# Attention and two feed-forward layers on one core: attention moved ahead of the first layer, which then runs in blocks of 1024 tokens by seven half-size products

## The reference

```python
# decaying linear attention: batch 4, 8 heads, 768 steps, head size 64
state = gamma * state + k[t] (x) v[t];   y[t] = scale * q[t] @ state
# first feed-forward (512 -> 2048 -> 512)
h = x @ w_in;  g = where(h > 0, h, exp(min(h, 0)) - 1);  x2 = g @ w_out
# second feed-forward (512 -> 1024 -> 512)
h = x2 @ w_in2; e = exp(h - max(h)); solu = h * e / (sum(e) + 1e-9)
out = (layer_norm(solu) * g_ln) @ w_out2
```

## Time and profile before

| | us |
|---|---|
| median of 3 runs | 891.65 |
| the profiled execution | 891.52 |
| its span in the trace | 889.7 |
| TensorE matmul busy | 880.3 (99%) |
| VectorE busy | 447.5 (50%) |
| ScalarE busy | 327.6 (37%) |
| GpSimd busy | 182.1 (20%) |

### The profile page before, as it was taken

The page is one execution under the profiler, slowest core; times in us unless marked ns, Lnnn a source line. Parts: engine busy times, 40 slices in busy tenths (PEclk is TensorE's granted clock), DMA queues, the critical chain, the costliest instruction groups (busy, mean ns, idle before and its releaser), DMA issues.

```text
span 889.7 us, 12234 instructions
## 1 busy us (share of the span) xinstructions
PE 880.3 (99%) x4998; PEld 718.4 (81%) x4998; DVE 447.5 (50%) x755; ACT 327.6 (37%) x524; POOL 182.1 (20%) x214
## 2 busy tenths in 40 slices
PE   8999999999999999999999999999999999999998
PEld 6788888888888888888888888888878888888886
DVE  4765433332333333332333233376797777777774
ACT  2654433233333333333333335553243333333332
POOL 4221102110111102110110015330334444444200
PEclk9999999999999999999999999999999999999999
DMA  9901131110301122110310021410211111111001
GB/s 346 407 26 45 48 93 50 48 49 1 122 21 48 48 65 78 48 48 1 97 46 1 1 71 48 144 47 1 71 49 47 48 48 48 48 48 48 24 25 47
DMA packets 34007, 57.81 MB, mean 65 GB/s; under 512 B 2848, under 2 KB 15392, under 8 KB 33952
## 3 DMA queue, kind: packets, MB, share of 16 engines
q1 hardware_dynamic: 33376, 56.70, 18.1%
q10 hardware_dynamic: 576, 0.33, 0.1%
HBM read 44.44 MB, written 12.58 MB: 64 GB/s over the span
## 4 chain that ended last, share of the span: by engine, by line
PE 95%; DVE 3%; issue 1%; DMA 0%; POOL 0%; ACT 0%; POOLq 0%; DVEq 0%; ACTq 0%
PE ps L508 11%; PE ps L512 10%; PE ps L486 10%; PE ps L509 10%; PE ps L487 10%; PE ps L492 10%; PE ps L609 4%; PE ps L611 4%; PE ps L610 4%; PE ps L520 4%; PE ps L522 4%; PE ps L521 4%; PE ps L440 3%; PE ps L471 3%; PE ps L595 2%; PE ps L468 1%
## 5 line engine op out<-in xcount | busy, mean ns | idle before, releaser
L734 DVE TENSOR_TENSOR g_lo<-e,g_hi 128x512 fp32r<-128x512 f32 x96 | 74.3, 774 | 168.3 <-ACT g_hi L967 168.1
L508 PE MATMUL ps<-g_hi,w_hi 128*128 128x512 f32 x384 | 154.0, 401 | 0.0
L486 PE MATMUL ps<-x_hi,w_hi 128*128 128x512 f32 x384 | 149.5, 389 | 0.7 <-ACT x_hi L924 0.7
L512 PE MATMUL ps<-g_lo,w_hi 128*128 128x512 f32 x384 | 149.9, 390 | 0.0
L509 PE MATMUL ps<-g_hi,w_lo 128*128 128x512 f32 x384 | 149.6, 390 | 0.0
L487 PE MATMUL ps<-x_hi,w_lo 128*128 128x512 f32 x384 | 149.4, 389 | 0.0
L967 ACT ACTIVATE g_hi<-e 128x512 fp32r<-128x512 f32 x96 | 60.7, 632 | 201.1 <-PE ps L512 185.2
L727 DVE SCALAR_TENSOR_TENSOR e<-e,ps 128x512 f32<-128x512 f32 x96 | 65.8, 685 | 133.6 <-ACT e L958 133.6
L355 POOL TENSOR_TENSOR tiles<-tiles,q_decay 128x512 f32<-128x512 f32 x23 | 31.1, 1354 | 385.1 <-DMA tiles<-units_dram 379.0
L956 ACT ACTIVATE e<-ps 128x512 f32<-128x512 f32 x96 | 57.3, 597 | 142.7 <-PE ps L492 141.9
L492 PE MATMUL ps<-x_lo,w_hi 128*128 128x512 f32 x384 | 102.6, 389 | 0.0
(11 more groups left out here) (84 smaller groups left out, 1177.0 us busy)
## 6 DMA issues: line engine op xcount, KB each, us to landing
tiles<-units_dram SPq DMA_DIRECT2D x46, 512.0 KB, 4.8
w_raw<-w_dram SPq DMA_DIRECT2D x32, 256.0 KB, 9.5
x_between<-x SPq DMA_DIRECT2D x24, 256.0 KB, 2.7
x_raw<-x_between SPq DMA_DIRECT2D x12, 512.0 KB, 3.6
out_dram<-y_sb SPq DMA_DIRECT2D x24, 256.0 KB, 2.0
w_raw<-w_out_dram SPq DMA_DIRECT2D x4, 512.0 KB, 4.1
w_raw<-w_in_dram SPq DMA_DIRECT2D x4, 512.0 KB, 5.6
tile<-units_dram SPq DMA_DIRECT2D x2, 512.0 KB, 10.5
```

The costliest lines, as they stand in the source:

```text
L486: nc.tensor.matmul(bank, hi, x_hi[:, j % 2, k, :], start=(k == 0), stop=False)
L508: nc.tensor.matmul(ps[:, 4 + m, :], hi, g_hi[:, f % 2, :], start=(f == 0), stop=False)
L512: last = nc.tensor.matmul(ps[:, 4 + m, :], hi, g_lo[:, f % 2, :], start=False, stop=(f == NF1 - 1))
L734: nc.vector.tensor_tensor(g_lo[:, f % 2, :], e[:, f % 2, :], g_hi[:, f % 2, :].bitcast(f32), ALU.subtract)\
```

## The change

Attention is taken out of the first layer's loop and put ahead of it, in 12 steps of two chunks each (two sequences at once). Each step of TensorE's loop issues the scores of the next step, then this step's key_values and values. q's decay stays on GpSimd, the state's decay moves there from VectorE, v's decay moves to ScalarE. For a sequence's first chunk q isn't scaled; its mask table holds the factor. 16 of the 24 chunks' results go to DRAM and are loaded again per block.

The first layer then has three blocks of 1024 tokens. Its up product takes weights in pairs of slices (24 units n in all), by seven products of 6 full matmuls each, the sums of weights on GpSimd (`sum_u`), those of x on VectorE (`sum_x`). Results of the second 512 tokens wait in a stash of 16 slices; after the eight units of a block, 15 `down` of that half follow each other. The weights of the up product are loaded and split again in each block. The second layer stays as it is, but for places in memory, PSUM banks, and where its weights are prepared. Line numbers in this section's diff are not those of the listing above.

```diff
 # TensorE
-            for j in range(NB):
-                up(j, 0)
-                up(j, 1)
-                for f in range(NF1):
...
+            scores(0)
+            for s in range(NS):
+                if 0 < s < NS - 1:
+                    scores(s + 1)
+                if s % NC < NC - 1:
+                    key_values(s)
+                values(s)
+                if s == 0:
+                    scores(1)
...
+            def scores(s):
+                slot = s % SLOTS
+                pe.wait_ge(k_in[slot], 16 * loads(s))
+                if s % NC > 0:
+                    pe.wait_ge(q_decayed, decays(s))
+                else:
+                    pe.wait_ge(q_in[slot], 16 * loads(s))
...
+            def up(n, i, bank, a, b, first):
...
+                for k in range(2):
+                    one = slice(k * P, (k + 1) * P)
+                    hi, lo = u_hi[n % 2][:, a, one], u_lo[n % 2][:, a, one]
+                    nc.tensor.matmul(bank, hi, x_hi[:, b, k, :], start=(first and k == 0), stop=False, skip_group_check=True)
+                    nc.tensor.matmul(bank, lo, x_hi[:, b, k, :], start=False, stop=False, skip_group_check=True)
+                    done = nc.tensor.matmul(bank, hi, x_lo[:, b, k, :], start=False, stop=(k == 1), skip_group_check=True)
...
+                up(n, P1, X, A11, B11, True)
...
+                up(n, P6, Y, S2, T2, True)
+                pe.wait_ge(p1_kept, n + 1)
+                up(n, P2, X, A12, B21, False)
...
+                up(n, P5, W, S1, T1, True)
+                pe.wait_ge(h_summed, sums(n, U2))
+                up(n, P7, Y, S3, T3, False)
+                between()
+                pe.wait_ge(h_summed, sums(n, U3))
+                up(n, P4, Y, A22, T4, False)
+                pe.wait_ge(h_summed, sums(n, H22))
+                up(n, P3, W, S4, B22, False)
...
+            for blk in range(NBLK):
+                for i in range(NFP):
...
+                        if i > 0:
+                            down(blk, 0, 2 * i - 1)
+                        elif blk > 0:
+                            down(blk - 1, 1, NF1 - 1)
+
+                    up_pair(n, between)
+                    down(blk, 0, 2 * i)
+                down(blk, 1, 0)
+                down(blk, 0, NF1 - 1)
+                for f in range(1, NF1 - 3):
+                    down(blk, 1, f)
 # GpSimd
+            for s in range(NS):
+                if (s + 1) % NC > 0:
+                    decay_q(s + 1)
+                if s % NC < NC - 1:
+                    decay_state(s)
+                if 2 <= s < 6:
+                    sum_u(0, s - 2)
+                if s >= 8:
+                    split_u_lo(0, 2 * (s - 8))
+                    if s < NS - 1:
+                        split_u_lo(0, 2 * (s - 8) + 1)
+            for n in range(1, NU):
+                for i in range(4):
+                    sum_u(n, i)
+                for i in range(7):
+                    split_u_lo(n, i)
...
+                nc.gpsimd.tensor_tensor(q, q, q_decay[:, :].unsqueeze(1).to_broadcast([P, 2, HH * C]), ALU.mult)\
+                    .then_inc(q_decayed, 1)
...
+            def decay_state(s):
+                pool.wait_ge(state_summed, kvs(s + 1))
 # VectorE
+                if s + 1 < NS:
+                    apply_mask(s + 1, 0)
+                    apply_mask(s + 1, 1)
+                if s % NC < NC - 1:
+                    sum_state(s)
+                if 4 <= s < 6:
+                    sum_x(0, 2 * (s - 4))
+                    sum_x(0, 2 * (s - 4) + 1)
+                if s >= 6:
+                    split_x_lo(0, s - 6)
...
+                dve.wait_ge(p1_kept, n + 1)
+                keep_sum(u2[:, :], n, U2, h21, Y, P6)
+                activate(e11, n, G11, X)
+                if blk == 0 and i < NFP - 1:
+                    wd_split_lo(2 * i + 2)
+                keep_sum(u3[:, :], n, U3, h21, Y, P7)
...
+                keep_sum(stash[:, 2 * i + 1, :], n, H22, u3[:, :], W, P5)
+                split_g_lo(down_no(blk, 0, 2 * i), e11)
...
+                activate(stash[:, 2 * i + 1, :], n, G22, stash[:, 2 * i + 1, :])
...
+                keep_sum(h21, n, H21, h21, Y, P4)
+                keep_sum(stash[:, 2 * i, :], n, H12, u2[:, :], W, P3)
+                activate(e21, n, G21, h21)
+                split_g_lo(down_no(blk, 0, 2 * i + 1), e21)
+                activate(stash[:, 2 * i, :], n, G12, stash[:, 2 * i, :])
 # ScalarE
+            for s in range(NS):
+                if s + 1 < NS:
+                    decay_v(s + 1)
+                if s >= 5:
+                    split_x_hi(0, s - 5)
+                if s in (5, 7):
+                    wd_split_hi((s - 5) // 2)
+                if s == 7:
+                    split_u_hi(0)
+                attended(s)
...
+            for s in range(NS - SLOTS, NS):
+                act.wait_ge(x_stored[s % SLOTS], 32 * stores(s))
+            for blk in range(NBLK):
+                for i in range(NFP):
+                    quadrants(NFP * blk + i)
...
+                act.wait_ge(part_done, products(n, P1))
...
+                nc.scalar.activation(p1[:, n % 2, :], X, ACT.Copy).then_inc(p1_kept, 1)
+                act.wait_ge(part_done, products(n, P2))
+                exponent(n, G11, X)
...
+                split_g_hi(down_no(blk, 0, 2 * i), e11)
+                if n + 1 < NU:
+                    split_u_hi(n + 1)
...
+                act.wait_ge(h_summed, sums(n, H22))
+                exponent(n, G22, stash[:, 2 * i + 1, :])
...
+                act.wait_ge(h_summed, sums(n, H21))
+                exponent(n, G21, p1[:, n % 2, :])
...
+                split_g_hi(down_no(blk, 0, 2 * i + 1), e21)
+                act.wait_ge(h_summed, sums(n, H12))
+                exponent(n, G12, stash[:, 2 * i, :])
 # SyncE
+                if s >= SLOTS:
+                    sp.wait_ge(scores_done, 2 * (s - SLOTS + 1))
+                sp.dma_start(k_sb[slot], part(1)).then_inc(k_in[slot], 16)
+                if s >= SLOTS:
+
+                    sp.wait_ge(att_done, s - SLOTS + 1)
+                sp.dma_start(q_sb[slot], part(0)).then_inc(q_in[slot], 16)
+                sp.dma_start(v_sb[slot], part(3)).then_inc(v_in[slot], 16)
```

More of the change, by code:

```diff
@@ new lines, in key_values @@
+            def key_values(s):
+                slot = s % SLOTS
+                pe.wait_ge(v_decayed, s + 1)
+                pe.wait_ge(kn_in[slot], 16 * kn_loads(s))
+                pe.wait_ge(state_summed, kvs(s))
+                for one in range(2):
+                    k, v = kn_sb[slot][:, one, :], v_sb[slot][:, one, :]
+                    for hh in range(HH):
+                        for h in (hh, HH + hh):
+                            c = slice(h * D, (h + 1) * D)
+                            last = nc.tensor.matmul(ps_kv[rows(h), one, hh, :], k[:, c], v[:, c], start=True, stop=True,
+                                                    skip_group_check=True)
+                last.then_inc(kv_done, 1)
@@ new lines, in values @@
+            def values(s):
+                slot = s % SLOTS
+                pe.wait_ge(v_decayed, s + 1)
+                pe.wait_ge(att_copied, 2 * s)
+                for one in range(2):
+                    pe.wait_ge(masked, 2 * s + 1 + one)
+                    for h in range(H):
+                        last = nc.tensor.matmul(ps_y(one, h), v_sb[slot][:, one, h * D:(h + 1) * D], A[s % 2][:, one, h, :],
+                                                start=(one == 0 and h % HH < 2), stop=(s % NC == 0), skip_group_check=True)
+                if s % NC > 0:
+                    pe.wait_ge(state_done, kvs(s))
+                    for one in range(2):
+                        for pair in range(2):
+                            for half in range(2):
+                                for odd in range(2):
+                                    h = HH * half + 2 * pair + odd
+                                    hh = h % HH
+                                    last = nc.tensor.matmul(ps_y(one, h), state[rows(h), s % 2, one, hh, :],
+                                                            q_sb[slot][rows(h), one, hh * C:hh * C + C],
+                                                            start=False, stop=True, skip_group_check=True)
+                last.then_inc(att_done, 1)
@@ L869, in _ @@
             solu_moments(1)
-            add(h2[:, 1, 0:512], 1, H21, p1[:, :], Y, P4)
+            add(h2[:, 1, 0:512], 1, H21, kept, Y, P4)
             solu_normalise(1)
```

1018 lines of the change are left out of this document (516 added, 502 removed).

## The result

The changed kernel takes 899.87 us, the median of four runs (897.25 to 900.58), against 891.68 (891.29 to 891.76) for the kernel before beside it. The ratio is 1.0087, interval 1.0066 to 1.0108: slower by 0.9%, outside the forecast range on its upper side. The profiled execution took 900.29, with a span of 898.5; its span forecast was 875.2, so 23.3 us are to be found.

What follows compares the result with a forecast made beforehand. TensorE was taken as the bound, waiting on GpSimd in front: attention 102.0, joint 2.3, matmuls 499.2, entry 1.5, second layer 265.2, clock 5, and 1.8 beside the span gave 877.0 us, 1.6% faster; range 857 to 893.

Steps and rivals of the forecast that it cites:

- the clock: Attention in front: TensorE's idle stretches drop it to half clock, four falls at under half of 3.0, 5 us in all.
- the chain through GpSimd's queue: Attention in front: scores, masks, state sum, state's decay, then q's decay make a 7.9 us cycle against TensorE's 6.36.
- the joint: Between attention and the first unit: ScalarE starts once the last store has landed, so TensorE waits about 2.3 us.
- the entry: Start of the second layer's products, where a copy stands behind ScalarE's splits: 1.5 us (0 to 4).
- rival B: Attention in front: the clock falls at every gap, 3.0 us in eight cycles, giving 896 us; chance 0.12.
- State decay 1.04, decay_q 2.3, low splits 0.76: Attention in front: prices from earlier trace rows, state's decay 1.04, q's 2.3 (2.0 to 2.7), two low splits 1.5 us.
- VectorE ... hidden as well: Attention in front: VectorE's 3.2 us and at most 2.5 more per step fit in the 7.9 us cycle, costing nothing.
- inside a unit: 0: First layer's 24 units: TensorE's 14.96 us cover VectorE's 7.8, ScalarE's 8.6 and GpSimd's 8.6, so no waits.
- the stash part: The stashed down products ending each block: splits and sums fit within 2.72 us per down, costing 0.
- rival C: First layer's units stall on sums and queue order: 889 us at 0.5 us a unit, 901 at 1.0; chance 0.12.
- Rival D: Attention in front: loads bound it at 346 GB/s, 7.5 us a step, giving 877 again; no chance of its own.
- Rival A: Attention in front: TensorE bounds it, 64.4 us instead of 81.1 from scores(2) and no clock loss, 855 us; chance 0.14.

Runs made afterwards that it cites:

- e3_fill: The changed kernel with matmuls that nobody reads filling TensorE's idle time ahead of eight steps' scores in front: 889.91 us, 0.9980 of the kernel before.
- e2_split_waits: The changed kernel with VectorE's low splits of x in steps 6 to 11 held until GpSimd has decayed the state: 897.02 us, 1.0060 of the kernel before.
- e8_scale: The changed kernel with q's decay first, four buffers, store wait moved, tail reordered, and last weights scaled by ScalarE, not GpSimd: 866.67 us (867.46 without that scaling edit).
- e11_three: The changed kernel with the edits of e2_split_waits, e3_fill and e4_joint together, GpSimd's queue order kept: 885.33 us, 0.9931 of the kernel before.
- e4_joint: The changed kernel with ScalarE's wait for attention's last stores moved from ahead of the units to the first high split of g: 895.41 us, 1.0049 of the kernel before.
- e1_q_ahead: The changed kernel with GpSimd scaling q for step s+2 ahead of decaying the state of step s: 881.22 us, 0.9885 of the kernel before.
- e5_slots: The changed kernel with the edits of e1_q_ahead and e4_joint, and four buffers instead of three for q, v and k: 870.59 us, 0.9762 of the kernel before.
- e10_p1_first: The changed kernel with q's decay first, four buffers, moved store wait, reordered tail, weights scaled on ScalarE, VectorE splits held, P1's copy first: 864.36 us, 0.9689.

## Why the prediction was wrong

Four terms of the sum failed, each by being too small: the clock, the chain through GpSimd's queue, the joint and the entry.

**"The clock": the term was mis-sized.** The forecast took four falls at a little under half of 3.0, 5 us. The profile has a fall behind seven gaps in front, at the joint and at the tail. e3_fill prices those in front at about 10. The argument against rival B, that late scores make TensorE denser and shrink the gap, failed: the half clock falls on scores and key_values, which feed the chain, so each gap brings the next. The rule of the Trainium skill that was weighed there (page "TensorE: Matmul & The Clock Gate", section "A second HAM failure mode: psum-queue depth-cycling"), short idles making the clock swing, had it right in kind: B's mechanism is what ran, at 10 and not at B's 24.

**"State decay 1.04, decay_q 2.3, low splits 0.76": contention left out.** The prices came from rows where the neighbour was mostly idle. Alone they hold (1.04, 2.34), but beside VectorE the decays take 1.95 and 2.79 to 3.27 in the changed kernel. Its two pairs of low splits in front take 1.85 and 1.40 for the 1.5 reckoned; over the whole first layer one takes 0.92 on average (L486) against 757 ns in the earlier trace rows. Without the clock attention ends at 107.6 (e3_fill), not 102: 5.6 us. Of these 3.6 are the state's decay in four steps, and that it is contention is shown (e2_split_waits), as it is for the tail (e8_scale). The remaining 2 us are read from the timeline only: longer neighbours, and q's load, which comes late in two steps (by 0.8 and 0.2 in e3_fill). Taking the state's decay out of the collision won only 0.6 of the 5.6 in e11_three, since other instructions then collided. "VectorE ... hidden as well" was true of its own time and false of what it did to GpSimd.

**"Joint 2.3".** It lost 6.0 with its half clock, 4.5 without it (e3_fill), 2.2 with the wait moved (e4_joint). The copies and the store were reckoned, their wait (1.96) too, but not the clock fall behind it, nor the start of the first unit, where TensorE waits 0.7 more for a copy and 0.8 for a sum.

**"Entry 1.5 (0 to 4)".** It lost 9.0. ScalarE's queue was looked at, but the wait came from VectorE, whose splits stood still beside GpSimd's weight scaling; then the clock fell once more.

**Right:** the account of matmuls and their pace (2202 full matmuls, 0.7 us lost in 460), "inside a unit: 0" and the stash part, so rival C was wrong; the second layer; and the chain through GpSimd's queue, by e1_q_ahead. **Rival D** was set aside as no case of its own; so it was with the order of the change, but one more buffer and the other order uncover it, and it then sets the front. **Rival A** could not come for the same reason: even e5_slots ends attention at 90.7, with a DMA share of 1.00 from 15 to 90 us. Its 64.4 us do not follow from the costs of the forecast either: eight steps of 6.36, one of 5.24 without key_values and the last 9.4 are 65.5.

In sum: 5.2 (clock in front, 10.2 for 5) + 5.6 (chain) + 3.7 (joint) + 7.5 (entry) + 0.7 (between) = 22.7 of 23.3; the other 0.6 is counting and rounding. Of these the clock at joint and entry is inside the two terms: 3.4 us at half speed each, 1.7 us apiece.

Against the kernel before, the removed matmuls gave their 32.6 us. There the opening, the attention in the loop and its insertions took 23.15 + 59.6 + 8 + 2.1 (what that account left open) = 92.9 us with TensorE busy. Now attention takes 117.8 and what is lost up to the second layer 16.2, 134.0 in all. So 41.1 us come back, 8.5 more than the 32.6. With the order of GpSimd's two decays turned the change wins 1.2%, with all the edits of e10_p1_first 3.1%.

## What to carry to other kernels

A dependent chain across engines that leaves TensorE idle for 2 us in every step can cost more than the idle: price the step with its next scores at half clock, and ask first whether the queue order can be turned (here that was worth 18.7 us). Work that is moved to GpSimd is priced beside the VectorE instructions that will then run, not by rows from a quiet stretch: here splits with two SBUF inputs held it for up to their own length, and its own instructions held the splits. Where work is taken together in front, add up its loads at once: 353 to 360 GB/s with all DMA engines busy (e10_p1_first, e5_slots) is the limit that showed once the chain was mended.

## What the runs showed of the hardware that was not expected

Products that nobody reads, in one gap fourteen of them and 3.19 us of TensorE's time, made the kernel faster: with 87 in all the front's granted clock was 0.99 to 1.00, and 10.0 us were won. The gaps of 2.0 to 4.2 us had 3.4 us at the lower level behind them, the last 6.8; the first, 2.5 us, had none. Nor had the wait of 2.0 us at the joint once the front before it was filled (e3_fill, granted 1.00), where the changed kernel had 3.4 us at half clock. By the times of their ends, VectorE and GpSimd stop each other rather than slow each other: 0.77 became 2.38, 1.04 became 1.95, and x's low split, 1.22 alone, became 2.91.
